# Attention before two MoE layers: fp32 on TensorE's row and column tiles, values stationary, in place of fp32r splits

## What is computed

```python
# q, k, v: (4, 8, 576, 64) float32
scores = scale * np.matmul(q, k.transpose(0, 1, 3, 2))
bias = slopes[:, None, None] * (-np.abs(rel))[None, :, :]
mask = (rel >= 0) & (rel < 128)
scores = np.where(mask, scores + bias[None], -1000000000.0)
scores = scores - np.max(scores, axis=-1, keepdims=True)
attn = np.exp(scores)
attn = attn / (np.sum(attn, axis=-1, keepdims=True) + 1e-09)
x = np.matmul(attn, v)      # then to (2304, 512)
# MoE layers: g(x @ w_in) @ w_out, twice, (2304, 512) -> 2048 -> 512
```

## Time and profile before

| | |
|---|---|
| median of 3 runs | 852.1 us (851.6 to 852.22) |
| the profiled execution | 850.05 us, span 848.2 us |
| TensorE (PE) busy | 841.0 us, 99% |
| weight loads (PEld) | 836.5 us, 99% |
| VectorE (DVE) | 711.7 us, 84% |
| ScalarE (ACT) | 538.4 us, 63% |
| GpSimd (POOL) | 116.5 us, 14%, all of it before 150 us |
| DMA | 186.45 MB, mean 220 GB/s |

### The profile page before, as it was taken

The page is one execution under the profiler, slowest core; times in us unless marked ns, Lnnn a source line. Parts: engine busy times, 40 slices in busy tenths (PEclk is TensorE's granted clock), DMA queues, the critical chain, the costliest instruction groups (busy, mean ns, idle before and its releaser), DMA issues.

```text
span 848.2 us, 15510 instructions
## 1 busy us (share of the span) xinstructions
PE 841.0 (99%) x5744; PEld 836.5 (99%) x5744; DVE 711.7 (84%) x982; ACT 538.4 (63%) x791; POOL 116.5 (14%) x82
## 2 busy tenths in 40 slices
PE   8999999999999999999999999999999999999998
PEld 8999999999999999999999999999999999999998
DVE  7888898786988966778998897989989789889794
ACT  7778787676776546767744556767556566765441
POOL 3788988000000000000000000000000000000000
PEclk9999999999999999999999999999999999999999
DMA  8978671667776347686764862587646643888822
GB/s 199 227 207 227 186 187 68 257 256 283 241 256 223 135 163 273 241 303 246 261 241 185 298 227 122 199 282 267 233 162 247 231 153 141 296 290 295 304 106 75
DMA packets 63257, 186.45 MB, mean 220 GB/s; under 512 B 7504, under 2 KB 14352, under 8 KB 59344
## 3 DMA queue, kind: packets, MB, share of 16 engines
q1 hardware_dynamic: 62896, 185.30, 64.0%
q10 hardware_dynamic: 288, 0.16, 0.1%
HBM read 113.09 MB, written 72.35 MB: 219 GB/s over the span
## 4 chain that ended last, share of the span: by engine, by line
PE 91%; DVE 5%; POOL 1%; issue 1%; ACT 0%; DMA 0%; SPq 0%; DVEq 0%; POOLq 0%
PE ps L1075 79%; PE ps L1043 5%; PE ps L1009 3%; PE ps L1022 3%; DVE arena L1755 1%; POOL qk_hi L895 1%; PE ps L1037 1%; DVE probs L1645 1%; POOL k_lo L892 1%; PE ps L1052 1%; DVE qk_hi L1613 0%; DVE raw_first L1714 0%; DVE g L1787 0%; DMA qk_raw<-qkT 0%; DVE raw_first L1709 0%
## 5 line engine op out<-in xcount | busy, mean ns | idle before, releaser
L1075 PE MATMUL ps<-arena,w_first 128*128 128x384 f32 x1764 | 328.4, 336 | 0.0
L1075 PEld LDWEIGHTS ps<-arena,w_first 128*128 128x128 f32 x1764 | 307.3, 188 | 1.0 <-DVE arena L1755 0.6
L1075 PE MATMUL ps<-arena,w_rest 128*128 128x384 f32 x1260 | 240.0, 336 | 0.1
L1075 PEld LDWEIGHTS ps<-arena,w_rest 128*128 128x128 f32 x1260 | 220.1, 188 | 0.8 <-DVE arena L1755 0.4
L1755 DVE TENSOR_TENSOR arena<-raw_first,arena 128x768 fp32r<-128x768 f32 (+1 forms) x114 | 148.8, 1319 | 74.4 <-ACT arena L1333 74.1
L1333 ACT ACTIVATE arena<-raw_first 128x768 fp32r<-128x768 f32 (+1 forms) x120 | 132.0, 1117 | 46.1 <-DVE raw_first L1714 39.0
L1075 PE MATMUL ps<-w_rest,arena 128*128 128x256 f32 x945 | 130.8, 280 | 0.2 <-DVE g L1858 0.2
L1075 PEld LDWEIGHTS ps<-w_rest,arena 128*128 128x128 f32 x945 | 119.5, 189 | 0.4 <-issue 0.4
L1075 PE MATMUL ps<-w_first,arena 128*128 128x256 f32 x567 | 86.2, 279 | 0.0
L1755 DVE TENSOR_TENSOR arena<-raw_rest,arena 128x1536 fp32r<-128x1536 f32 (+1 forms) x48 | 71.3, 1486 | 7.1 <-ACT arena L1333 7.0
L1333 ACT ACTIVATE arena<-raw_rest 128x1536 fp32r<-128x1536 f32 (+1 forms) x48 | 60.9, 1269 | 22.4 <-PE ps L1075 20.2
(11 more groups left out here) (125 smaller groups left out, 971.0 us busy)
## 6 DMA issues: line engine op xcount, KB each, us to landing
gd<-g SPq DMA_DIRECT2D x24, 1536.0 KB, 6.1
raw_rest<-gd SPq DMA_DIRECT2D x32, 768.0 KB, 5.1
wst<-w_pairs SPq DMA_DIRECT2D x32, 512.0 KB, 5.7
raw_first<-gd SPq DMA_DIRECT2D x16, 768.0 KB, 6.0
yd<-ust SPq DMA_DIRECT2D x6, 1536.0 KB, 6.3
qk_raw<-qkT SPq DMA_DIRECT2D x30, 288.0 KB, 3.9
wd<-ust SPq DMA_DIRECT2D x4, 1536.0 KB, 8.8
raw_first<-yd SPq DMA_DIRECT2D x4, 1536.0 KB, 7.2
```

What stands on the lines that cost most here:

```text
L1075: last = nc.tensor.matmul(to, stationary, moving, start=start and n == 0, stop=n == len(steps) - 1, skip_group_check=True)
```

## The change

The attention stage is written anew; the MoE part is the same but for the hand-over between the two.

- Scores are one fp32 matmul per block. The two heads of a pair stand in the upper and the lower 64 partitions of one tile `qk`, as do their queries and keys, so head 0 uses the upper 64 rows of the array and head 1 the lower 64; the tail's result also goes to 64 columns each. The matmuls of the two heads alternate. All splitting and rounding of q and k goes, and so do half of the loads.
- A pair's blocks 2 and 3 are the first group (items 0 to 3), the rest the second (items 4 to 8). There is one set of four score banks.
- The exponential gives the row's sum (`accum_out`), VectorE inverts the sums of a group, and GpSimd multiplies each block's probabilities by them before they are transposed.
- In the value product the values are stationary (64 columns; head 0 on the array's first 64 columns, head 1 on the last) and the transposed probabilities move. The result is the transposed output of both heads, which VectorE copies to `x_pairs` in one instruction (`copy_x`). The transposes of the output and their copies go.
- ScalarE keeps all copies of transposed probabilities, four a pair.
- The split of S2 moves from GpSimd to VectorE, behind a copy of an output and two weight splits; the splits of A11 and S1 on GpSimd move up between the scalings of pairs 13 and 15. The first duo waits for four marked banks.
- SP issues one load of operands a pair, one store and two loads of values.

```diff
-        def split_head(head):
-            slot = head % SPLIT_RING
-            pool.wait_ge(qk_rounded, head - 2)
-            nc.gpsimd.tensor_tensor(k_lo[:, slot], keys(qk_raw, head), f32(keys(qk_hi, head)),
-                                    ALU.subtract).then_inc(qk_split[slot], 1)
...
+        def scale_probs(q, group):
+            pool.wait_ge(sums_inverted, 2 * q + group + 1)
+            for item in ((4, 5, 6, 7, 8) if group else (0, 1, 2, 3)):
+                at = prob(q, item)
+                nc.gpsimd.tensor_scalar(at, at, inverse[:, q % PROB_RING, item:item + 1], None,
+                                        ALU.mult).then_inc(probs_scaled, 1)
...
+        for q in range(PAIR_COUNT):
+            scale_probs(q, 0)
+            if q == PAIR_COUNT - 1:
+                split_operand(S1)
+            scale_probs(q, 1)
...
+        def wide_scores(q):
...
+                pe.wait_ge(scores_biased, made(q - 1, 3))
+            for blk in (2, 3):
+                for e in range(2):
+                    last = nc.tensor.matmul(score_bank[e][:, (blk - 2) * BAND:(blk - 1) * BAND], queries(q, e, blk),
+                                            keys(q, e, (blk - 1) * P, BAND), start=True, stop=True)
...
+        def other_scores(q):
...
+                pe.wait_ge(scores_biased, made(q - 1, 8))
+            for blk in (1, 0):
...
+            for part in range(2):
+                for e in range(2):
+                    last = nc.tensor.matmul(score_bank[2 + part][ROWS[e], 3 * P:3 * P + TAIL_HALF], queries(q, e, 4),
+                                            keys(q, e, SEQ - TAIL_KEYS + part * TAIL_HALF, TAIL_HALF), start=True, stop=True)
...
+        def weigh_values(q):
+            h = 2 * q % HEADS
+            for e in range(2):
+                pe.wait_ge(pt_copied[e], 2 * q + 2)
+            pe.wait_ge(v_in[q % BATCH_PAIRS], 32 * (q // BATCH_PAIRS + 1))
+            wait_past(pe, x_copied, q)
+            for blk in range(4):
+                width = BAND if blk < 3 else P
+                for e in range(2):
+                    nc.tensor.matmul(ps[ROWS[e], out_bank, blk * P:blk * P + width], v_sb[:, h + e, blk],
+                                     probs_t[:, q % 2, e, (2 * blk + 1) * P:(2 * blk + 1) * P + width],
+                                     start=blk == 0, stop=blk == 3, skip_group_check=True)
...
+        for q in range(PAIR_COUNT):
+            wide_scores(q)
+            other_scores(q)
...
+                transpose_wide(q - 1)
+                if q > 1:
+                    weigh_values(q - 2)
+                transpose_others(q - 1)
...
+        def exponentials(q, items):
+            for item in items:
+                act.wait_ge(scores_biased, made(q, item))
+                at = prob(q, item)
+                nc.scalar.activation(at, at, ACT.Exp, bias=neg_max[:, q % PROB_RING, item:item + 1], scale=-1.0,
+                                     accum_out=inverse[:, q % PROB_RING, item:item + 1]).then_inc(probs_made, 1)
...
+        for q in range(PAIR_COUNT):
+            exponentials(q, (0, 1, 2, 3))
+            if q:
+                copy_transposed(q - 1, 0)
+            exponentials(q, (4, 5, 6, 7, 8))
+            if q:
+                copy_transposed(q - 1, 1)
...
+        def invert_sums(q, group):
+            at = inverse[:, q % PROB_RING, 4:9] if group else inverse[:, q % PROB_RING, 0:4]
+            dve.wait_ge(probs_made, made(q, 8 if group else 3))
+            nc.vector.tensor_scalar(at, at, 1e-9, None, ALU.add).then_inc(sums_guarded, 1)
+            dve.wait_ge(sums_guarded, 2 * q + group + 1)
+            nc.vector.reciprocal(at, at).then_inc(sums_inverted, 1)
+        def copy_x(q):
+            pair = q % BATCH_PAIRS
+            dve.wait_ge(pv_done, 2 * (q + 1))
+            wait_past(dve, x_stored[pair], 16 * (q // BATCH_PAIRS))
+            nc.vector.tensor_copy(x_pairs[:, pair], out_banks[:, 0:SEQ]).then_inc(x_copied, 1)
...
+        for q in range(PAIR_COUNT):
+            bias_scores(q, (0, 1, 2, 3))
+            invert_sums(q, 0)
+            bias_scores(q, (4, 5, 6, 7, 8))
+            if q > 1:
+                copy_x(q - 2)
+            if q == PAIR_COUNT - 2:
+                sum_operand(0, S1)
+            if q == PAIR_COUNT - 1:
+                split_first_weights(1)
+            invert_sums(q, 1)
+        sum_operand(0, S2)
+        copy_x(PAIR_COUNT - 2)
+        split_half_weights(1)
...
+        split_operand(0, S2)
+        copy_x(PAIR_COUNT - 1)
```

More of the change, by code:

```diff
@@ L250, in wait_past @@
             engine.wait_ge(semaphore, count)
-    def pair_end(q):
-        return max(m for m, (pair, _) in enumerate(ORDER) if pair == q)
-    def pair_at(m, lag):
-        return next((q for q in range(PAIR_COUNT) if pair_end(q) + lag == m), None)
-    def group_of(m):
-        return next(i for i, (_, last) in enumerate(GROUPS) if last >= m)
-    def prob_place(m, i):
-        d = ORDER[m][1] - 1
-        return probs[:, d, i], 2 * d + i
-    def was_before(m):
-        q, d = ORDER[m]
-        return ORDER.index((q - 1, d)) if q else -1
@@ L295, in piece_queries @@
-    def piece_queries(tile, e, first, rows):
-        return piece(tile, 0, first)[rows, 1] if e == 0 else all_queries(tile, 1, rows)
-    def piece_lo(e, first):
-        return k_lo[:, e, 0:FIRST_COLS] if first else k_lo[:, e, FIRST_COLS:SEQ]
-    def splits(head):
-        use = head // SPLIT_RING
-        return 2 * use + 2 - (1 if head % SPLIT_RING == 1 else 0) if head >= 0 else 0
-    def last_use(head):
-        return max(m for m, (q, d) in enumerate(ORDER) if q == head // 2 and
-                   (d == 0 or any(e == head % 2 for e, _ in ITEMS[d])))
@@ L311, in loaded, with made @@
[L311 to L325 removed]
+    def made(q, item):
+        return len(ITEMS) * q + item + 1
@@ new lines, in weigh_values @@
+        def weigh_values(q):
+            h = 2 * q % HEADS
+            for e in range(2):
+                pe.wait_ge(pt_copied[e], 2 * q + 2)
[3 more added lines that the diff above has]
+                width = BAND if blk < 3 else P
+                for e in range(2):
+                    nc.tensor.matmul(ps[ROWS[e], out_bank, blk * P:blk * P + width], v_sb[:, h + e, blk],
+                                     probs_t[:, q % 2, e, (2 * blk + 1) * P:(2 * blk + 1) * P + width],
+                                     start=blk == 0, stop=blk == 3, skip_group_check=True)
+            for piece in range(2):
+                for e in range(2):
+                    last = nc.tensor.matmul(ps[ROWS[e], out_tail_bank, 0:TAIL], v_sb[:, h + e, 3 + piece],
+                                            probs_t[:, q % 2, piece, e * TAIL:(e + 1) * TAIL],
+                                            start=piece == 0, stop=piece == 1)
+                    if piece:
+                        last.then_inc(pv_done, 1)
@@ L1375, in copy_d @@
             wait_past(act, c12_done, D - 1)
-            if D == 0:
-                for head in range(2 * PAIR_COUNT - SPLIT_RING, 2 * PAIR_COUNT):
-                    act.wait_ge(qk_split[head % SPLIT_RING], splits(head))
             nc.scalar.activation(d1(D, pos), d_bank(D, pos), ACT.Copy).then_inc(d_copied, 1)
@@ L1661, in copy_pair_tail, with bias_scores @@
-        def copy_pair_tail(q):
-            pair = q % BATCH_PAIRS
-            dve.wait_ge(pair_tail_transposed, q + 1)
-            for half in range(2):
-                rows = slice(half * TAIL, (half + 1) * TAIL)
-                last = nc.vector.tensor_copy(x_pairs[rows, pair, 4 * P:SEQ], xt_bank[rows, rows])
-            last.then_inc(pair_tail_copied, 1)
+        def bias_scores(q, items):
+            for item in items:
+                pair = q % BATCH_PAIRS
+                if q < BATCH_PAIRS:
+                    dve.wait_ge(bias_made, 3 * q + (3 if item == TAIL_ITEM else ITEMS[item][0] + 1))
+                dve.wait_ge(scores_ready, 4 * q + (4 if item >= TAIL_ITEM else 2))
+                wait_past(dve, probs_transposed, 4 * (q - PROB_RING) + (4 if item >= TAIL_ITEM else 2)
+                          if q >= PROB_RING else 0)
+                dve.sem_inc(dve_gate, 1)
+                if item == TAIL_ITEM:
+                    to, bias = (ap.rearrange("p (t n) -> p t n", t=2) for ap in (prob(q, item), bias_tail[:, pair]))
+                else:
+                    e, blk = ITEMS[item]
+                    to, bias = prob(q, item), bias_sb[:, 2 * pair + e, BAND - (P if blk == 0 else BAND):BAND]
+                nc.vector.tensor_tensor_reduce(out=to, in0=scores_of(item), in1=bias, scale=-SCALE, scalar=3.0e38,
+                                               op0=ALU.add, op1=ALU.min,
+                                               accum_out=neg_max[:, q % PROB_RING, item:item + 1]).then_inc(scores_biased, 1)
```

621 lines of the change are left out of this document (178 added, 443 removed).

## The result

| | before | after |
|---|---|---|
| median of 4 runs each | 851.85 us (851.58 to 852.22) | 861.56 us (861.02 to 862.48) |
| profiled execution, span | 850.05, 848.2 | 861.25, 859.3 |
| TensorE busy | 841.0 (99%) | 822.5 (96%) |
| GpSimd busy | 116.5 (14%) | 142.4 (17%) |
| last biased score | 137.3 | 132.9 |

The changed kernel is slower: ratio 1.0115, 95% interval 1.0097 to 1.0132. "End of the first duo" is here the start of the first matmul that reads `w_rest` behind it; what follows takes the same time in both kernels (690.5 and 690.4 us to the end of the span).

What follows compares the result with a forecast made beforehand. TensorE was taken to bound the attention stage at 8.08 us a pair; 6.5 a pair gave -23.6 us, the hand-over +4.5, sum -19.1, so 833.0 us. Forecast's own range 824 to 844, stated range 822 to 868.

Steps and rivals of the forecast that it cites:

- rival A: TensorE in the attention stage: the two heads' tiles don't run side by side; 862 us (854 to 870), chance 0.17.
- Step (4): GpSimd, per pair: splits go, nine scalings come; 3.5 to 6.0 us, taken 4.5; under 6.2 nobody waits.
- Rival C: Elementwise engines in the attention stage are dearer, 7.3 us a pair, +12; 845 us (840 to 853), chance 0.12.
- Step (1): TensorE, per pair: 5.8 us with tiles side by side, 6.6 with five dear changes of tile shape, against 8.08.
- Step (2): ScalarE, per pair: nine exponentials with row sums and four copies, 6.15 us; besides, 7.8 us of work once in the stage.
- Step (3): VectorE, per pair: biased scores, two inverses and the copy of the output, 4.4 us; it waits for ScalarE before each inverse.
- Steps (5) to (7): Attention stage's loop, start and end: 6.5 us a pair against 8.08, last biased score at 113.7 us against 137.3.
- Step (6): Start of the attention stage: no split stands before the first score; the first exponential starts at 6.4 us.
- Step (7): End of the attention stage: last biased score at 113.7 us against 137.3, a gain of 23.6 us.
- Step (8): Hand-over into the MoE part: last bias to first duo's end takes 23.7 to 26.8 us against 20.2, +4.5 us.
- D: TensorE's clock falls to 1.2 GHz, a pair takes about 12 us; about 905 us, chance 0.06.
- B: TensorE: only one kind of tile runs side by side, 7.2 to 8.1 us a pair; 846 to 857 us, chance 0.08.

Runs made afterwards that it cites:

- the run with S1 on VectorE: The changed kernel with the low half of operand S1 made by VectorE after the last inverses, not by GpSimd between its last scalings; 859.04 us, ratio 1.0084.
- the one-row-tile run: Kernel without scaling, with the second head's score matmuls of blocks 0 to 3 repeating the first head's on its rows; 849.37 us, ratio 0.9984.
- the run with the heads' order: Kernel without scaling, with scores of blocks 0 to 3 and values done first for one head, then the other, instead of alternating; 843.02 us, ratio 0.9898.
- the kept-busy run: The changed kernel with matmuls of no use into a free bank during TensorE's waits at the hand-over; 859.99 us, ratio 1.0106.

## Why the prediction was wrong

The forecast was 833, and faster; the kernel took 861.56. Against the profiled execution the miss is 861.25 - 831 = 30.2 us: 19.2 at the last biased score (132.9, forecast 113.7) and 11.1 behind it (36.0, forecast 24.9). The time lies in the stated range, and at 862, the price of rival A; that is chance, as A's mechanism, tiles that don't run side by side, isn't there.

- **Step (4), GpSimd, failed,** and with it the sign. The prediction named its mark in advance, a GpSimd line as releaser of most transposes. Scaling was priced by a memset and by the two-input subtraction, 0.42 to 0.74 us for 256 columns, and 4.5 us a pair taken. It took 0.92 us on the mean, outside both ends; nine take 7.3 us, not 3.5 to 6.0. With its other work GpSimd passes the 6.2 us "under which nobody waits" by 2 us. Little of the 0.92 is time in which VectorE holds it up: in the run with S1 on VectorE the starts of two wide scalings lay 1.15 us apart beside VectorE's subtraction, and 0.90 while VectorE was idle. The 0.90 is GpSimd's own; why a scaling costs more than a subtraction stays open. The error was to treat the subtraction's row as a dear end because it reads more. Rival C had the mechanism, but by the same dear end, so at 7.3 us a pair, where 8.3 came out (five from 60.20 to 101.51).
- **Step (1), TensorE, was right.** 5.8 to 6.6 us a pair were forecast; 6.14 came out where TensorE was the bound. Two cycles a column and tiles side by side stand. The change of shape costs what the dear end said at two places of five, where TensorE's loads wait "[0.17 <-issue]" (L868 and L919); the other three show no such wait, and the whole sum came out 0.3 above the 5.8 without any, not 0.8. The rule of the Trainium skill ("TensorEngine Tiling (Array Packing)", Key Properties) that changing the tiling mode drains the array agrees with the number at these two.
- **Step (2), ScalarE, was right.** 6.15 us a pair forecast, 6.37 with its once-only work when it was the bound. The read of a row sum costs 0.09 (exponentials start every 0.49 in place of 0.40); its own row says 189 ns, as it overlaps its neighbours.
- **Step (3), VectorE**: the sum held, except that its inverse waits for GpSimd (below).
- **Steps (5) to (7)** follow from 6.5 us a pair. With GpSimd out of the way the last biased score came at 112.8, 0.9 us from the forecast, but by two errors that cancel. Step (6) had the first exponential at 6.4; it came at 10.17 in the change and at 10.04 without scaling, since ScalarE makes the tail's bias ahead of it and waits for its load:
```profile
9.90 0.36 ACT L1113 ACTIVATE bias_tail<-distance 128x192 f32<-128x192 f32 x1 [3.94 <-DMA distance<-bias_table]
```
  Step (7) had 107.3 us from there to the last biased score; 102.8 came out, since it adds 7.8 us of once-only work to pairs of 6.5, where twelve pairs took 6.50 on the mean with most of that work in them (27.12 to 105.10).
- **Step (8), the hand-over, failed by 11.1 us.** Without scaling it was 26.5 us, inside the 23.7 to 26.8 of the step, though 1.6 of it came from a low clock that the step doesn't have (product 6 1.86 us and the values 2.74, where 1.28 and 1.74 are the prices at 1.00). The 9.5 us above that went with the scalings. 8.6 of them lie ahead of product 6 (18.1 us from the last biased score, 9.5 without scaling): the last groups of scalings end 14 us behind the last biased score, 1.8 us of that by S1's split between them and 2.3 by VectorE's subtractions beside the last five; the rest wasn't taken apart further. The other 1.0 is the low clock behind product 6's start, 2.5 us here and 1.6 without scaling.
- **The rivals.** A was refuted by the one-row-tile run, and for the column tiles by the timeline: the sixteen value instructions, 3584 columns, would take 3.0 us one after the other at two cycles a column, and the next group starts 1.56 us behind their start. D didn't come: the granted clock was 1.00 from 50 to 125 us with TensorE at 78 to 83% busy. But the clock did fall at the hand-over, and to 0.67 and 0.66 from 20 to 25 and from 40 to 45 us, which the prediction had at 1.00 throughout. The fall at 40 us cost nothing: with 1.00 from 25 to 50 us, in the run with S1 on VectorE, the last biased score came at 133.1, not before 132.9. B fell with the 6.14 us. The sign came from C's mechanism, at a price that no rival had.

## What to carry to other kernels

Work moved to an engine has to be priced by an operation of its own kind on that engine; where there is none, the nearest row is no bound, and the question is from what price on this engine becomes the bound, here 6.2 / 9 = 0.69 us a scaling, over all widths, where 7.3 / 9 = 0.81 was measured. The engine's other work, 0.8 to 2.4 us a pair here, lowers that point further. If the unknown price lies near it, the forecast should carry it as its main rival, and the operation is best moved or shared: 839.0 us with all of it on VectorE, and 829.6 with it shared, a shorter hand-over and one copy moved, in place of 861.6, with the same matmuls. A wait of TensorE on the critical path can be dearer than its length, since what follows may run at the low clock (2.5 us here).

## What the runs showed of the hardware

- **VectorE waits for GpSimd even for five columns.** An inverse's guard, 128x5, took 0.77 us on the mean in the changed kernel (the one before, of ten columns and out of PSUM, 0.17), at worst:
```profile
126.25 1.78 DVE L1438 TENSOR_SCALAR inverse<-inverse 128x5 f32<-128x5 f32 x1
```
It ends with GpSimd's subtraction (125.70 + 2.31 = 128.01). With the scaling on VectorE the same guard took 0.16 on the mean. The Trainium skill ("SBUF — State Buffer", Who interferes with whom) says that VectorE and GpSimd share a pair of ports as an exclusive lock, and that a VectorE operation with two inputs in SBUF contends with a GpSimd one that reads SBUF; the weight splits agree (4.21 against 1.82).
- **The wait goes both ways.** GpSimd's 128-column scaling took 1.68 us beside VectorE's weight splits and 0.60 with VectorE idle.
- **Tiles are served out of the program's order,** as the run with the heads' order showed (L920 at 76.58, L915 still at 76.79). The Trainium skill ("TensorE: Matmul & The Clock Gate", Part 3) says that matmuls are never reordered; here the measurement decides.
- **The clock isn't set by the wait's length alone.** After the same two waits near 130 us (1.35 and 1.14 or 1.15) it was granted 0.59 in the change (132 to 135 us) and 1.00 in the run with S1 on VectorE.
- **One thing stays open.** Near the end TensorE, full in both, started 91 matmuls in ten microseconds in the change and 87 in the kept-busy run, of the same code. First the change, then that run:
```profile
829.30:839.30 10.00, 10.00 (x91) 10.00 (x90) 8.19 (x5) 5.33 (x8) 0.00 (x0) 1.00 0.43 159
```
```profile
829.00:839.00 10.00, 10.00 (x87) 10.00 (x86) 6.55 (x4) 5.08 (x7) 0.00 (x0) 1.00 0.33 122
```
It is worth about 2 us (2.8 in one run): behind the first duo seven profiled executions, both kernels' among them, took 690.3 to 690.7 us, the other six 692.3 to 693.2. It need not go by kernel: thirteen executions of the kernel before, timed beside the run with one row tile, lie five at 849.8 to 850.3 us and eight at 851.7 to 852.5. No experiment asked for its cause. Effects of 2 us are therefore read at the end of the first duo as well.
